# Attention: the low parts of q and k are made by VectorE for even heads and by GpSimd for odd heads

## The reference

```python
scale = 1.0 / np.sqrt(q.shape[-1])
scores = scale * np.matmul(q, k.transpose(0, 1, 3, 2))
thresh = np.max(scores, axis=-1, keepdims=True) - tau
scores = np.where(scores >= thresh, scores, -1000000000.0)
scores = scores - np.max(scores, axis=-1, keepdims=True)
attn = np.exp(scores)
attn = attn / (np.sum(attn, axis=-1, keepdims=True) + 1e-09)
return np.matmul(attn, v).astype(np.float32)
```

## Time and profile before

| what | value |
|---|---|
| median of 3 runs | 1318.75 us (1318.21 to 1320.85) |
| the profiled execution, its own time | 1318.25 us |
| its span, first to last instruction | 1316.5 us |
| TensorE busy | 95% of the span |
| GpSimd, VectorE, ScalarE busy | 43%, 47%, 41% of the span |
| attention, about | the first 368 us of the span |

### The profile page before, as it was taken

One profiled execution on the slowest core, in us unless ns is written; L12 is line 12 of the kernel. 1 busy time (PEld: TensorE's weight loads), 2 busy tenths in 40 slices (PEclk: granted clock), 3 DMA queues, 4 the chain that ended last, 5 costly groups with the idle time before them and its releaser, 6 DMA issues.

```text
span 1316.5 us, 20225 instructions
## 1 busy us (share of the span) xinstructions
PE 1245.1 (95%) x7678; PEld 1135.2 (86%) x7678; DVE 620.3 (47%) x1243; ACT 536.8 (41%) x962; POOL 568.2 (43%) x412
## 2 busy tenths in 40 slices
PE   4999999999885999999999999999999999999998
PEld 4899989989864889999899998998999999999997
DVE  6888888888745521212112121215544535444433
ACT  3787777877742333333323333333212112111211
POOL 2999999999810354343525344354411101000000
PEclk9999999999986999999999999999999999999999
DMA  5545554554430153433424243344221102000000
GB/s 164 131 120 135 143 139 120 144 135 128 139 82 24 47 162 104 136 122 103 128 96 143 92 132 111 114 154 132 91 73 49 32 1 73 16 0 24 16 1 25
DMA packets 71810, 124.45 MB, mean 95 GB/s; under 512 B 11952, under 2 KB 30640, under 8 KB 71728
## 3 DMA queue, kind: packets, MB, share of 16 engines
q1 hardware_dynamic: 57856, 88.22, 23.8%
q0 software_dynamic: 6080, 19.93, 4.8%
q10 hardware_dynamic: 7792, 15.21, 3.1%
HBM read 82.43 MB, written 19.92 MB: 78 GB/s over the span
## 4 chain that ended last, share of the span: by engine, by line
PE 73%; POOL 10%; issue 5%; DMA 5%; ACT 3%; DVE 3%; SPq 0%; ACTq 0%; POOLq 0%; DVEq 0%
PE h_ps L683 32%; PE y_ps L701 10%; PE y_ps L702 10%; PE y_ps L700 10%; POOL probs_lo L1276 6%; PE o_acc L541 3%; DMA k_parts<-k_ones 2%; DMA q_lo<-k_parts 2%; PE t_ps L661 2%; POOL k_parts L1281 2%; PE ring L511 2%; PE ring L512 1%; POOL region_a L1287 1%; PE ring L525 1%; PE ring L524 1%
## 5 line engine op out<-in xcount | busy, mean ns | idle before, releaser
L683 PE MATMUL h_ps<-x_hi,region_a 128*128 128x384 f32 (+1 forms) x1408 | 343.9, 317 | 4.8 <-DVE x_lo L1168 4.3
L683 PEld LDWEIGHTS h_ps<-x_hi,region_a 128*128 128x128 f32 x1408 | 246.5, 189 | 11.5 <-DVE x_lo L1168 5.2
L1276 POOL TENSOR_TENSOR probs_lo<-probs,probs_hi 128x576 fp32r<-128x576 f32 x160 | 226.7, 1428 | 29.7 <-ACT probs_hi L778 29.7
L683 PE MATMUL h_ps<-x_lo,region_a 128*128 128x384 f32 (+1 forms) x704 | 221.2, 314 | 0.0
L1178 DVE SCALAR_TENSOR_TENSOR h_lo<-h_ps,h_hi 128x256 fp32r<-128x256 f32 (+1 forms) x128 | 62.8, 491 | 310.3 <-ACT h_hi L871 291.2
L874 ACT ACTIVATE h_hi<-act_out 128x384 fp32r<-128x384 f32 (+1 forms) x112 | 53.7, 479 | 312.4 <-DVE act_out L1189 305.9
L700 PE MATMUL y_ps<-region_b,h_hi 128*128 128x512 f32 x448 | 175.8, 392 | 1.4 <-DVE h_lo L1195 1.4
L701 PE MATMUL y_ps<-region_b,h_hi 128*128 128x512 f32 x448 | 176.6, 394 | 0.0
L702 PE MATMUL y_ps<-region_b,h_lo 128*128 128x512 f32 x448 | 176.4, 394 | 0.0
L1262 POOL TENSOR_TENSOR region_b<-stage,region_b 128x1024 fp32r<-128x1024 f32 x40 | 95.8, 2398 | 142.3 <-ACT region_b L759 142.1
L871 ACT ACTIVATE h_hi<-h_ps 128x256 fp32r<-128x256 f32 (+1 forms) x128 | 56.0, 437 | 239.2 <-PE h_ps L683 234.9
(11 more groups left out here) (198 smaller groups left out, 2398.8 us busy)
## 6 DMA issues: line engine op xcount, KB each, us to landing
stage<-in_moe_w SPq DMA_DIRECT2D x56, 512.0 KB
qk_raw<-in_qk SPq DMA_DIRECT2D x32, 320.0 KB, 3.3
expert_rows<-rows_out ACTq DMA_DIRECT2D x8, 768.0 KB, 3.8
v_nat<-in_v SPq DMA_DIRECT2D x16, 320.0 KB, 3.7
k_ones<-q_hi SPq DMA_DIRECT2D x32, 160.0 KB, 2.9
q_lo<-k_parts SPq DMA_DIRECT2D x32, 160.0 KB, 2.4
q_hi<-q_hi SPq DMA_DIRECT2D x32, 160.0 KB, 2.4
k_parts<-k_ones SPq DMA_DIRECT2D x32, 160.0 KB, 2.9
```

The source lines that it names most:

```text
L683: mm = pe.matmul(h_ps[:, c % 2, 0:width], wt, x[kind][:, cc, :], start=(n == 0), stop=(n == 3 * C - 1))
L1276: pool.tensor_tensor(probs_lo[:, m % 4, :], probs[:, m % 4, :], probs_hi[:, m % 4, :].bitcast(F32), ALU.subtract).then_inc(lo_done, 1)
```

## The change

The low parts of heads 0, 2, 4, ... 30 are made by VectorE, those of heads 1, 3, ... 31 by GpSimd. Before, VectorE made those of heads 0 and 1, and GpSimd those of 2 to 31. The place in the slot stays: behind line 970 on VectorE, behind line 1276 on GpSimd. The two semaphores are renamed and counted by parity.

```diff
         def parts_split(eng, heads):
 
-            wait(eng, qk_lo_first, min(heads, LO_FIRST))
-            wait(eng, qk_lo_done, heads - LO_FIRST)
+            wait(eng, qk_lo_even, (heads + 1) // 2)
+            wait(eng, qk_lo_odd, heads // 2)
...
                 g = split_in(i, c)
-                if g is not None and has(i, g, NH, U) and head(i, g) < LO_FIRST:
+                if g is not None and has(i, g, NH, U) and g % 2 == 0:
                     s = g % U
                     wait(dve, qk_hi_done, head(i, g) + 1)
                     dve.tensor_tensor(k_parts[:, s, :], qk_raw[:, s // 2, s % 2, :], q_hi2[:, s, :].bitcast(F32),
-                                      ALU.subtract).then_inc(qk_lo_first, 1)
+                                      ALU.subtract).then_inc(qk_lo_even, 1)
...
                 g = split_in(i, c)
-                if g is not None and has(i, g, NH, U) and head(i, g) >= LO_FIRST:
+                if g is not None and has(i, g, NH, U) and g % 2 == 1:
                     wait(pool, qk_hi_done, head(i, g) + 1)
                     pool.tensor_tensor(k_parts[:, g % U, :], qk_raw[:, g % U // 2, g % 2, :],
-                                       q_hi2[:, g % U, :].bitcast(F32), ALU.subtract).then_inc(qk_lo_done, 1)
+                                       q_hi2[:, g % U, :].bitcast(F32), ALU.subtract).then_inc(qk_lo_odd, 1)
```

More of the change, by code:

```diff
@@ L107, in build @@
         v_in = [sem(f"v_in{i}") for i in range(2)]
-        qk_hi_done = sem("qk_hi_done"); qk_lo_done = sem("qk_lo_done"); qk_lo_first = sem("qk_lo_first")
+        qk_hi_done = sem("qk_hi_done"); qk_lo_even = sem("qk_lo_even"); qk_lo_odd = sem("qk_lo_odd")
         parts_in = [sem(f"parts_in{i}") for i in range(2)]
@@ L311, in build @@
         rows = lambda c: P if c % NT < FULL else TAIL
-        LO_FIRST = 2
         def parts_split(eng, heads):
-            wait(eng, qk_lo_first, min(heads, LO_FIRST))
-            wait(eng, qk_lo_done, heads - LO_FIRST)
+            wait(eng, qk_lo_even, (heads + 1) // 2)
+            wait(eng, qk_lo_odd, heads // 2)
         def span(n, size):
```

## The result

The change makes the kernel slower: median 1326.38 us (1322.78 to 1328.49, 10 runs) against 1319.41 us (1316.47 to 1320.85, 10 runs of before beside it), a ratio of 1.0048 with a 95% interval of 1.0039 to 1.0058, or 6.3 us (5.1 to 7.7). The prediction was 6.4 us slower.

The account below looks back on a forecast made before the run. The prediction took a loop of waits, not a full engine, to bound the kernel. Start +2.0, heads 4, 8, ... +4.9, heads 6, 10, ... 0 and transfers -0.5 gave +6.4 us on 1318.25, so 1324.7 (1325 against the runs), range 1315.5 to 1335.

Parts of the forecast that it names:

- The loop: Steady attention runs on a loop of waits; GpSimd's k_parts subtraction lies outside it, so its 1.571 us is no term.
- The start, +2.0: Head 2's low parts, now VectorE's, come 2.75 us later; 0.75 comes back at head 3's wait: +2.0 us.
- no clock enters the sum: Granted clock is 9 tenths or more in all but two of 40 slices, both behind attention, so it adds nothing.
- Heads 4, 8, ... 28, 7 x 0.70 = +4.9: VectorE's subtraction and GpSimd's weight part block each other at SBUF: 0.70 us a head in seven heads, +4.9 us.
- the sign given for it: In heads 4, 8, ... TensorE's wait ahead of line 540 grows from 0.65 or so to 1.3 us.
- Heads 6, 10, ... 30, 0: VectorE's subtraction starts in GpSimd's idle 0.74 us; GpSimd's low part ends 0.38 us later, before TensorE wants it: 0.
- the cover: In heads 6, 10, ... GpSimd's delayed low part ends 0.04 us before TensorE wants it; without this, 0.38 us each.
- Earlier transfers, -0.5: Even heads' low parts come 2.2 us or more earlier, removing some TensorE waits for k_parts: -0.5 us, at most -3.7.
- The first rival: GpSimd's relief counts, its low part behind the subtraction being 1.57 us earlier: faster, 1311 to 1315 us; chance 0.14.
- The second: Rival: no disturbance where it matters, GpSimd not held, only the start left: 1319.8 us, down to 1317; chance 0.15.
- The third: Rival: VectorE not let in between GpSimd's back-to-back instructions in heads 4, 8, ...: 3.3 us a head, 1343 us; chance 0.15.

Follow-up runs that it names:

- b1: GpSimd's subtraction of heads 4, 6, ... 30 cut to the first 64 of 640 columns, nothing moved to VectorE, against the kernel before: ratio 1.0005.
- a3: Only the low parts of heads 6, 10, ... 30 moved to VectorE, against the kernel before: ratio 1.0003, no difference.
- a4: Low parts of heads 5, 7, ... 31 moved to VectorE, all others as in the kernel before: ratio 0.9988, 1.6 us faster.
- a1: Only heads 1 and 2 change engines (1 to GpSimd, 2 to VectorE), against the kernel before: ratio 1.0018, 2.4 us slower.
- c1: Low parts of heads 4, 6, ... 30 on VectorE, heads 0, 1 and 2 as in the kernel before: ratio 1.0028, 3.7 us slower.
- a2: Only the low parts of heads 4, 8, ... 28 moved to VectorE, against the kernel before: ratio 1.0034, 4.5 us slower.
- b2: Heads 4, 6, ... 30 on VectorE as a reduction with one SBUF input in place of the subtraction, start as before, against the kernel before: ratio 1.0000.
- c3: Heads 5, 7, ... 31 on VectorE, GpSimd's weight part in slots 8 and 13 in place of 5 and 10, against the kernel before: 1.0162, 21 us slower.
- c2: Heads 5, 9, ... 29 on VectorE, GpSimd's weight part in slots 7 and 12 in place of 5 and 10, against the kernel before: 0.9929, 9.4 us faster.

## Why the prediction was right

**The loop.** Right for the even heads: a subtraction behind the low part of the next head's first tile is in no loop. b1 shows it by itself, and a3. It is not so for all heads: a4 and the runs with later weights got GpSimd's time back in heads 5, 9, ... (above).

**The start, +2.0.** Measured alone 2.4 us (1.2 to 3.7), so the size was right, but three of its steps were off, and that they came out even is luck. First, line 418's transfer was later than worked out (3.36 us, not 2.75; VectorE came to the subtraction at 22.85, not 22.26), but the queue went on 2.38 us behind it and not 3.76 as before, so TensorE was 2.02 us late. Second, head 3's low parts do get later: they stand on GpSimd behind a low part of the probabilities, which is late with all the rest, and start at 32.30 in place of 29.72. TensorE's wait ahead of head 3's scores fell from 0.75 to 0.34 us, so 0.4 us came back and not 0.75. ScalarE's exponentials of tile 4 start 2.39 us later than before (35.24 against 32.85); the 2.96 us at tile 14 have head 4's long lap in them.

Third, "no clock enters the sum" does not hold for the start. The profile after has the stretch at clock 0.51 shown above, and a1's has one from 30.4 to 33.7 us; the one before has none there. Over whole executions the granted clock is 0.9845 on average with the change (10 executions) and 0.9847 in a1 (10), against 0.9868 for the kernel before beside a1 (26) and 0.9870 in c1, which has the change without its start. a1's two executions at 0.987 took 1319.28 and 1319.72 us, where the kernel before at 0.987 took 1319.31 on average; its slowest, 1324.76, had 0.983. So a part of the 2.4 us goes with the lower clock. How large a part is not shown, nor that the later transfer brings the lower clock: the profiles of a2 and a4, with the start as before, have one such stretch too (27.2 to 30.5 and 28.9 to 32.2 us).

**Heads 4, 8, ... 28, 7 x 0.70 = +4.9.** Measured 0.61 us a lap (0.59 in head 4's), 4.2 for seven; a2 gave 4.5. The size was right, and that the loss comes from the two engines' holding each other up is shown by b2. One step was incomplete. TensorE's recorded wait in six of the seven heads is not for GpSimd but for VectorE, through the maxima and the ring's place (line 523), and the sign given for it, a wait of 1.3 us ahead of line 540, did not come: there is none in head 12, and 1.05 us in head 16. I had taken VectorE's delay as covered by TensorE's wait for GpSimd. The two are nearly of one length: in head 12 GpSimd's low part of tile 45 ends at 131.82 and line 540 starts at 131.91, and in the other five there is 0.09 to 0.10 us between them too. So the sum did not suffer, and taking away only one of the two delays would have given back 0.1 us a head at most, an estimate from these rows.

The rule of the Trainium skill ("SBUF — State Buffer", section "Who interferes with whom"), that the first to issue holds the shared interface for its whole instruction, agrees with the trace in both directions: VectorE's 1.66 us in head 4, where GpSimd starts first, and the 1.66 us of GpSimd's low part in heads 6, 10, ..., where VectorE does. For the 1.98 and 1.97 us in the heads with equal starts the order can't be read. A wait for one instruction covers head 12; in c3 VectorE waited for the rest of one and for two more, 4.11 us in all.

**Heads 6, 10, ... 30, 0.** Right: a3 at +0.4 us (-0.8 to 1.6), and 0.81 us for each of VectorE's subtractions. GpSimd's low part beside it grew by 0.23 us (1.66 in place of 1.43), within the cover.

**Earlier transfers, -0.5.** Too small to be seen. That about half of the 7.3 us belongs to even heads was right: 3.65 us, ahead of heads 4, 6, 10, 14 and 22. But making the low parts of even heads earlier did little to it. Ahead of heads 6, 10, 14 and 22 TensorE's weight loads waited 3.35 us before and 3.04 after.

**The first rival** fell with b1, for the heads that the change moves; on heads 5, 9, ... its mechanism is there. **The second** fell with the rows of head 12 and with a2. **The third** did not come in this kernel; c3 shows that its mechanism exists.

**What stays open.** Why VectorE is let in between GpSimd's weight part and the next low part (the change, six of seven heads), and not between two low parts (c3, six heads). The runs differ in the kind of instruction ahead and in how early the next one could start; none of them separates the two. Open too are the share of the clock in the start's 2.4 us, and whether it is the second SBUF input or the kind of operation that made the difference in b2.

## What to carry to other kernels

Before work is moved off the busiest engine, find the loop of waits that sets the period and ask whether the operation is inside it: 17.4 us less on an engine that was 92% busy were worth nothing here, and an operation of 1.29 us that is made 16 times, moved by two slots each time, was worth 3.2 us. When a two-input operation goes to VectorE beside a busy GpSimd, look at what GpSimd runs at that moment: in a gap it cost nothing (a3), beside a GpSimd operation VectorE lost the rest of that operation and GpSimd 0.6 us of the next. Put on the second engine those pieces behind which the first one is late for somebody (one head in four in c2), not every second one. And when a change moves the first matmuls, compare the granted clock of that stretch and of whole executions before a loss there is put down to a transfer.

## What the runs showed of the hardware

- A VectorE subtraction with two inputs in SBUF beside GpSimd's took 1.64 to 1.98 us in place of 0.82, and where GpSimd was the one held up its instruction took 1.97 in place of 1.29; a VectorE reduction of the same length with one SBUF input took 0.81 us at the same place.
- Beside three GpSimd instructions back to back VectorE's subtraction took 4.11 us: it was not let in at two boundaries between them.
- A transfer of 160 KB issued 3.36 us later, at a time with fewer others ahead of it, let the queue go on 1.4 us faster (2.38 against 3.76 us behind its issue; the DMA engines' mean share was 0.36 from 24 to 26 us, and 0.95 from 20 to 22 us before).
- TensorE's granted clock was 0.51 for 3.3 us at the start of attention in four of the kernels' profiles (the change, a1, a2, a4), in each in a stretch of another place between 25.5 and 33.7 us, and 1.00 there in the others. The 40 slices of the page show 9 tenths in both cases.
